# Reordering the prologue of a fused attention and feed-forward kernel: first loads, first scores and output-weight splits

## The reference

```
scale = 1/8
pp  = softmax(scale * p @ k^T) @ v         # 32 packed rows per head
x   = softmax(scale * q @ pp^T) @ pp       # back to 576 rows, heads side by side: [4608, 512]
xn  = x / rms(x) * rms_g
x   = (silu(xn @ w_gate) * (xn @ w_val)) @ moe_w_out     # inner size 1536
y   = (((x @ w1) * (x @ w2)) @ w3) @ w_out               # inner size 1024, all fp32
```

## Time and profile before

| | |
|---|---|
| runs | 1411.97, 1412.69, 1413.43 us (median 1412.69) |
| profiled execution | 1412.07 us, of which the span of the core is 1410.3 us |
| TensorE matmuls | 1386.3 us busy, 98% of the span |
| VectorE, ScalarE, GpSimd | 605.7, 406.9, 141.4 us busy |
| chain that ended last | PE 95%, DVE 3%, ACT 1%, issue 1% |
| granted TensorE clock | mean 0.999 |

### The profile page before, as it was taken

How to read it: one execution, slowest core, us unless ns; L and a number is a source line. 1 busy time by engine, 2 the same in 40 slices (tenths; PEclk the granted TensorE clock), 3 DMA queues, 4 the chain that set the end, 5 groups by cost and what they waited for, 6 DMA issues and landing times.

```text
span 1410.3 us, 22634 instructions
## 1 busy us (share of the span) xinstructions
PE 1386.3 (98%) x9688; PEld 1194.8 (85%) x9688; DVE 605.7 (43%) x1095; ACT 406.9 (29%) x803; POOL 141.4 (10%) x137
## 2 busy tenths in 40 slices
PE   7989999999999999999999999999999999999999
PEld 5679899898898998988989988888888888888887
DVE  3657556565565565655655632212212111212111
ACT  4253342433423424334233422111111111111111
POOL 0100100001001000010012030220202020202000
PEclk9999999999999999999999999999999999999999
DMA  9882451533424515323024130101011010100000
GB/s 332 233 314 82 129 163 41 196 106 93 165 86 128 163 39 197 107 92 131 18 69 167 47 107 0 60 0 60 0 60 45 16 60 0 60 0 30 0 30 30
DMA packets 59155, 129.13 MB, mean 92 GB/s; under 512 B 3504, under 2 KB 12720, under 8 KB 57264
## 3 DMA queue, kind: packets, MB, share of 16 engines
q1 hardware_dynamic: 59056, 127.70, 27.6%
HBM read 106.69 MB, written 20.99 MB: 91 GB/s over the span
## 4 chain that ended last, share of the span: by engine, by line
PE 95%; DVE 3%; ACT 1%; issue 1%; DMA 0%; SPq 0%; DVEq 0%; ACTq 0%
PE psum L586 9%; PE psum L584 9%; PE psum L585 9%; PE psum L546 8%; PE psum L565 7%; PE psum L567 7%; PE psum L566 7%; PE psum L547 7%; PE psum L548 7%; PE psum L606 5%; PE psum L605 5%; PE psum L604 5%; PE psum L513 3%; PE psum L500 1%; PE psum L526 1%; PE psum L467 1%
## 5 line engine op out<-in xcount | busy, mean ns | idle before, releaser
L546 PE MATMUL psum<-a_hi,m_hi 128*128 128x288 f32 x768 | 240.7, 313 | 0.4
L565 PE MATMUL psum<-g_hh,wo_hi 128*128 128x288 f32 x768 | 227.4, 296 | 4.5 <-DVE g_res L921 2.6
L547 PE MATMUL psum<-a_lo,m_hi 128*128 128x288 f32 x768 | 226.7, 295 | 0.0
L548 PE MATMUL psum<-a_hi,m_lo 128*128 128x288 f32 x768 | 226.3, 295 | 0.0
L567 PE MATMUL psum<-g_hh,wo_lo 128*128 128x288 f32 x768 | 226.0, 294 | 0.0
L566 PE MATMUL psum<-g_hl,wo_hi 128*128 128x288 f32 x768 | 225.9, 294 | 0.0
L1012 DVE TENSOR_TENSOR b_h<-b_s,psum 128x512 f32<-128x512 f32 x72 | 49.5, 688 | 408.9 <-PE psum L586 408.9
L584 PE MATMUL psum<-xh,w_hi 128*128 128x512 f32 x576 | 224.1, 389 | 0.0
L585 PE MATMUL psum<-xl,w_hi 128*128 128x512 f32 x576 | 224.1, 389 | 0.0
L586 PE MATMUL psum<-xh,w_lo 128*128 128x512 f32 x576 | 224.1, 389 | 0.0
L546 PEld LDWEIGHTS psum<-a_hi,m_hi 128*128 128x128 f32 x768 | 144.4, 188 | 50.6 <-issue 46.6
(11 more groups left out here) (109 smaller groups left out, 1737.2 us busy)
## 6 DMA issues: line engine op xcount, KB each, us to landing
w_in<-in_w_gate SPq DMA_DIRECT2D x24, 1024.0 KB, 5.3
w_in<-in_w_val SPq DMA_DIRECT2D x24, 1024.0 KB, 5.3
kT<-in_kT SPq DMA_DIRECT2D x8, 1152.0 KB, 7.7
v_sb<-in_v SPq DMA_DIRECT2D x8, 1152.0 KB, 7.2
qT<-in_qT SPq DMA_DIRECT2D x16, 576.0 KB, 3.8
y_scratch<-g_res SPq DMA_DIRECT2D x16, 576.0 KB, 3.2
x_raw<-y_scratch SPq DMA_DIRECT2D x9, 1024.0 KB, 7.6
out<-b_res SPq DMA_DIRECT2D x8, 1024.0 KB, 5.2
```

The costliest lines, as they stand in the source:

```text
L546: nc.tensor.matmul(in_ps[which], hi, a2_hi[:, t, par, :], start=par == 0, stop=False)
L547: nc.tensor.matmul(in_ps[which], hi, a2_lo[:, t, par, :], start=False, stop=False)
L548: last = nc.tensor.matmul(in_ps[which], lo, a2_hi[:, t, par, :], start=False, stop=par == 1)
L565: nc.tensor.matmul(out_ps[m], hi, hh[:], start=f == 0, stop=False)
```

## The change

All of it concerns the prologue and the first steps of the main loop:
1. Loads: the first piece of w_out and w3 is one chunk instead of two and is loaded ahead of pT and kT of batch 0 (pieces of 1, 1, 2, 2, 2 chunks). The second half of w3 comes ahead of batch 1's pT and kT. The output weights come in pieces of 1, 3, 4, 4 chunks, and `store_wf(1)` stands after the second piece.
2. TensorE: fuse(0,0) ahead of the first scores; fuse(0,1) and fuse(0,2) ahead of both AT items, which stand side by side.
3. S1(0,1) and AT(0,1) write banks 0 and 1 and don't wait for the item before them to be copied out.
4. The lo parts of w_out (eight subtractions) move from VectorE to GpSimd.
5. S1(1,0) and S1(1,1) move from the end of the prologue to places after fuse(0,7) and fuse(1,1).
6. ScalarE's and VectorE's orders follow: ScalarE copies both AT items before fuse_split(0,3); VectorE does fuse_split(0,2) before sums1, `wf_evict(0)` after fuse_split(1,2), and `wf_evict(1)` after M(0,3).

```diff
 FIRST_ITEMS = [("S1", 0, 0), ("S1", 0, 1), ("AT", 0, 0), ("AT", 0, 1), ("PV", 0, 0), ("PT", 0, 0), ("S2", 0, 0), ("S2", 0, 1),
-               ("Z", 0, 0), ("Z", 0, 1), ("SS", 0, 0), ("M", 0, 0), ("M", 0, 1), ("M", 0, 2), ("M", 0, 3),
-               ("S1", 1, 0), ("S1", 1, 1)]
+               ("S1", 1, 0), ("Z", 0, 0), ("S1", 1, 1), ("Z", 0, 1), ("SS", 0, 0), ("M", 0, 0), ("M", 0, 1), ("M", 0, 2), ("M", 0, 3)]
+FUSE_LOADS = [slice(0, 1), slice(1, 2), slice(2, 4), slice(4, 6), slice(6, 8)]
+WO_LOADS = [slice(0, 1), slice(1, 4), slice(4, 8), slice(8, 12)]
...
+def first_bank(kind, a, part):
+
+    return 0 if kind in ("S1", "AT") and (a, part) == (0, 1) else 6
...
+            load_fuse(0, 0)
             load_kp(0)
-            load_fuse(0, 0)
             load_fuse(0, 1)
+            load_fuse(0, 2)
             load_v(0)
-            load_fuse(0, 2)
             load_fuse(0, 3)
+            load_fuse(0, 4)
             load_q(0, 0)
             sp.dma_start(gcol[:], g_d).then_inc(g_loaded, 16)
             load_q(0, 1)
+            for i in range(len(FUSE_LOADS)):
+                load_fuse(1, i)
             load_kp(1)
-            for i in range(4):
-                load_fuse(1, i)
...
-            for i in range(3):
-                rows = slice(4 * i, 4 * i + 4)
+            for i, rows in enumerate(WO_LOADS):
                 sp.dma_start(wo_raw[:, rows, :], wo_v[:, rows, :]).then_inc(wo_loaded[i], 16)
-                if i == 0:
+                if i == 1:
                     store_wf(1)
...
+            for c in range(FC2):
+                pool.wait_ge(wout_hi_ready, c + 1)
+                nc.gpsimd.tensor_tensor(wout_lo[:, c, :], wout_raw[:, c, :], wout_hi[:, c, :].bitcast(F32),
+                                        ALU.subtract).then_inc(wout_lo_ready, 1)
...
             pe.wait_ge(const_ready, 3)
+            fuse(0, 0)
             item("S1", 0, 0)
             item("S1", 0, 1)
-            fuse(0, 0)
             fuse(0, 1)
+            fuse(0, 2)
             item("AT", 0, 0)
-            fuse(0, 2)
             item("AT", 0, 1)
             fuse(0, 3)
...
             fuse(0, 7)
+            item("S1", 1, 0)
             fuse(1, 0)
             item("Z", 0, 0)
             fuse(1, 1)
+            item("S1", 1, 1)
             fuse(1, 2)
...
-            item("S1", 1, 0)
-            item("S1", 1, 1)
             for b in range(B):
...
+            fuse_split(0, 0)
             item("S1", 0, 0)
             item("S1", 0, 1)
-            fuse_split(0, 0)
             fuse_split(0, 1)
             exp1(0, 0)
             exp1(0, 1)
             fuse_split(0, 2)
             item("AT", 0, 0)
+            item("AT", 0, 1)
             fuse_split(0, 3)
-            item("AT", 0, 1)
             fuse_split(0, 4)
...
-            fuse_split(1, 0)
-            fuse_split(1, 1)
+            for c in range(3):
+                fuse_split(1, c)
             wf_evict(0)
+            item("S1", 1, 0)
             exp2(0, 1)
-            for c in range(2, FC2):
+            fuse_split(1, 3)
+            fuse_split(1, 4)
+            item("S1", 1, 1)
+            for c in range(5, FC2):
                 fuse_split(1, c)
...
             act.wait_ge(wf_stored[0], 16)
-            item("S1", 1, 0)
-            item("S1", 1, 1)
             wo_split(0)
...
             def fuse_split(half, c):
-                if half == 0:
-                    dve.wait_ge(wout_hi_ready, c + 1)
-                    nc.vector.tensor_tensor(wout_lo[:, c, :], wout_raw[:, c, :], wout_hi[:, c, :].bitcast(F32),
-                                            ALU.subtract).then_inc(wout_lo_ready, 1)
...
             fuse_split(0, 1)
+            fuse_split(0, 2)
             sums1(0)
-            for c in range(2, 7):
+            for c in range(3, 7):
                 fuse_split(0, c)
...
-            wf_evict(0)
             item("Z", 0, 0)
             fuse_split(1, 2)
+            wf_evict(0)
             fuse_split(1, 3)
...
             a2_split(0, 0)
+            item("M", 0, 3)
             wf_evict(1)
-            item("M", 0, 3)
             wo_split(0)
```

More of the change, by code:

```diff
@@ L65, in item_numbers, with load_of @@
     return number
+def load_of(loads, c):
+    return next(i for i, rows in enumerate(loads) if c < rows.stop)
+def first_bank(kind, a, part):
+    return 0 if kind in ("S1", "AT") and (a, part) == (0, 1) else 6
 def before(b, t, f):
@@ L191, in build @@
         w_in_loaded = [sem(f"w_in_loaded{i}") for i in range(W_BUFS)]
-        wout_loaded = [sem(f"wout_loaded{i}") for i in range(4)]
-        w3_loaded = [[sem(f"w3_loaded{h}{i}") for i in range(4)] for h in range(2)]
+        wout_loaded = [sem(f"wout_loaded{i}") for i in range(len(FUSE_LOADS))]
+        w3_loaded = [[sem(f"w3_loaded{h}{i}") for i in range(len(FUSE_LOADS))] for h in range(2)]
         wout_hi_ready, wout_lo_ready = sem("wout_hi_ready"), sem("wout_lo_ready")
         w3_hi_ready, w3_lo_ready = sem("w3_hi_ready"), sem("w3_lo_ready")
-        wo_loaded = [sem(f"wo_loaded{i}") for i in range(3)]
+        wo_loaded = [sem(f"wo_loaded{i}") for i in range(len(WO_LOADS))]
         fuse_done, wf_act, wf_dve, wf_stored = sem("fuse_done"), sem("wf_act"), sem("wf_dve"), [sem(f"wf_stored{i}") for i in range(2)]
@@ L295, in load_fuse @@
             def load_fuse(half, i):
-                rows = slice(2 * i, 2 * i + 2)
+                rows = FUSE_LOADS[i]
                 if half == 0:
@@ L458, in item @@
                 n = number[kind, a, part]
-                if n:
+                bank = first_bank(kind, a, part)
+                if bank == 0:
+                    n -= 1
+                if n > 0:
                     pe.wait_ge(xy_free, n)
@@ L466, in item @@
                             rows, cols = slice(DH * par, DH * (par + 1)), slice(NP * c, NP * (c + 1))
-                            last = nc.tensor.matmul(xy[par][cols, 0:HALF], pT[rows, cols], kT[rows, c, HALF * part:HALF * (part + 1)],
+                            last = nc.tensor.matmul(psum[cols, bank + par, 0:HALF], pT[rows, cols], kT[rows, c, HALF * part:HALF * (part + 1)],
                                                     start=True, stop=True)
@@ L471, in item @@
                     for j in range(NT):
-                        last = nc.tensor.transpose(xy[j // 3][0:TP, j % 3 * P:(j % 3 + 1) * P], sc[:, part, TP * j:TP * (j + 1)], ident[:])
+                        last = nc.tensor.transpose(psum[0:TP, bank + j // 3, j % 3 * P:(j % 3 + 1) * P], sc[:, part, TP * j:TP * (j + 1)], ident[:])
                 if kind == "PV":
@@ L660, in item @@
                     full(act, "S1", a, part)
-                    nc.scalar.copy(sc[:, :, HALF * part:HALF * (part + 1)], psum[:, 6:8, 0:HALF]).then_inc(xy_free, 1)
+                    bank = first_bank(kind, a, part)
+                    nc.scalar.copy(sc[:, :, HALF * part:HALF * (part + 1)], psum[:, bank:bank + 2, 0:HALF]).then_inc(xy_free, 1)
                 if kind == "AT":
                     full(act, "AT", a, part)
-                    nc.scalar.copy(a1T[:, part, :].rearrange("p (a n) -> p a n", a=2), psum[0:TP, 6:8, 0:3 * P]).then_inc(xy_free, 1)
+                    bank = first_bank(kind, a, part)
+                    nc.scalar.copy(a1T[:, part, :].rearrange("p (a n) -> p a n", a=2), psum[0:TP, bank:bank + 2, 0:3 * P]).then_inc(xy_free, 1)
                 if kind == "PV":
@@ L699, in fuse_split @@
                 if half == 0:
-                    act.wait_ge(wout_loaded[c // 2], 16)
+                    act.wait_ge(wout_loaded[load_of(FUSE_LOADS, c)], 16)
                     nc.scalar.copy(wout_hi[:, c, :], wout_raw[:, c, :]).then_inc(wout_hi_ready, 1)
-                act.wait_ge(w3_loaded[half][c // 2], 16)
+                act.wait_ge(w3_loaded[half][load_of(FUSE_LOADS, c)], 16)
                 nc.scalar.copy(w3_hi[half][:, c, :], w3_raw[half][:, c, :]).then_inc(w3_hi_ready, 1)
@@ L706, in wo_split @@
                 act.wait_ge(fuse_done, 2)
-                act.wait_ge(wo_loaded[f // 4], 16)
+                act.wait_ge(wo_loaded[load_of(WO_LOADS, f)], 16)
                 nc.scalar.copy(wo_hi[:, f, :], wo_raw[:, f, :]).then_inc(wo_hi_ready, 1)
```

## The result

| | before | after |
|---|---|---|
| runs | 20, 1411.86 to 1413.43 us | 20, 1413.58 to 1418.76 us |
| median | 1412.46 us | 1416.72 us |
| ratio, after to before | | 1.0028, 95% interval 1.0021 to 1.0035 |
| profiled execution | 1412.07, span 1410.3 | 1413.70, span 1411.9 |
| start of outof(0) in it | 84.88 | 86.16 |

The changed kernel is slower by 0.28%, 4.3 us in the median. Two things stand out. The profiled execution is only 1.6 us slower than before, and it is one of the fastest of its kind: the kernel before spreads over 1.6 us, the changed one over 5.2. So the result has two halves, what the profile shows in every execution, and what differs between them.

A forecast was written before the change was run, and what follows sets the result against it. PE is busy 98% of the span, so only its waits and slow stretches can be won. Front +3.5, middle -1.35, loop start -3.3 sum to -1.15; one clock fall of 1.4 makes +0.3: 1413.0 us, range 1408.5 to 1416.5.

The forecast's parts named there:

- step 1: First loads: w_out chunk 0 lands at 4.2 us, w3 chunk 0 at 5.1, kT 1.35 later than before.
- step 2: Front splits: POOL and DVE subtractions exclude each other, one turn each; the exposed pair takes 2.0 us instead of 1.35.
- The case where POOL keeps two in a row: W_out chunks 3 and 4, ready at once: POOL does both subtractions first, making DVE's w3_lo(3) 1.3 us later; kept for the range.
- step 3: Front up to PV: first step 5.9 us earlier, PV 3.2 late; with chunk 5's exposed split, +3.5 us.
- Gap 1: PE's wait for w3_lo(1) ahead of fuse(0,1): 3.3 us.
- gap 2: PE's new wait for w3_lo ahead of fuse(0,3), behind the two AT items: 3.75 us.
- step 4: Middle, up to M(0,3): waits for w3_lo and w3b_lo vanish, -2.65; batch 1's two S1 come in, +1.3; sum -1.35 us.
- step 5: Loop start, M(0,3) to outof(0): S1 waits go, outof(0) then waits for DVE's g_hl; -3.3 us.
- the clock: Slower rival: long slow start or fall at gap 1, plus falls at gap 2 and outof(0); 1415 to 1417 us, chance 0.20.
- Exclusion doesn't bite: Faster rival: POOL and DVE overlap in the front, PV only 0.95 late; sum -3.7, 1409.0 us, chance 0.22.
- the start isn't earlier: Rival: first small pieces land at 6 instead of 5.1, times to PV move by 0.9; +1.2, 1413.9 us, chance 0.08.
- It does nothing: Rival: new gaps repay the earlier start, no clock fall; -1.15, 1411.5 us, chance 0.5 together with the main case.

The follow-up runs named there:

- the kernel with fillers: Changed kernel plus extra matmuls after into(0) and into(1) and ahead of fuse(0,1) and fuse(0,3), filling PE's waits: 1412.17 us, ratio 0.9999.
- maxima moved: Kernel with the front as before and the rest of the change, plus maxima and bias of batch 1's first scores moved ahead of M(0,0): 1409.71 us.
- the old front: Changed kernel with loads, order, banks and splits up to PV as in the kernel before: 1409.36 us, ratio 0.9979.

## Why the prediction was right or wrong

I had forecast 1413.0 with 1408.5 to 1416.5, and gave slower by over 0.2% a chance of 0.17, the smallest. The measured ratio is just that, and the median of 1416.72 lies at the end of the range, 0.2 beyond it. For the profiled execution, 0.6 under the median before, the same sum gave 1412.3, and it took 1413.70. That it came so near is partly luck: loads that were 1.0 earlier than reckoned covered most of the 1.4 by which the middle failed. For the median the side was wrong.

**First loads (step 1): earlier than reckoned.** ACT's first cast started at 3.35, not 4.2; w_out chunk 0 landed 2.6 us after its issue. fuse(0,0) started at 5.97 instead of 7.0.

**Exclusion (step 2): right.** w3_lo took 1.36 in the median beside POOL and 0.68 without. At chunks 3 and 4 the two subtractions of each engine took 2.96 on POOL and 3.04 on DVE together, one turn each, as I took it. The Trainium skill ("SBUF — State Buffer", "Who interferes with whom") states that the second blocks until the first finishes, which this agrees with; that each waits for one at most was my reading, since it doesn't say whose turn comes next. The case where POOL keeps two in a row didn't occur in the front.

**Front (step 3): right but for the clock.** Gap 1 was 3.33 (3.3 forecast), the wait for chunk 2 0.48 (0.3), gap 2 3.34 (3.75). PE's slow start was longer than reckoned: the matmuls of fuse(0,0) are 0.43 apart up to 10.37, and the step took 5.03 instead of 4.3. With no fall PV starts at 29.24 in the kernel with fillers; 30.1 less the 1.0 of the loads is 29.1.

**Middle (step 4): this step failed.** I forecast -1.35. PV moved by +4.34 (26.89 to 31.23), and M(0,3) by +4.64 (72.92 to 77.56), so this stretch took 0.3 more. Of that, 0.2 is the exposed split of chunk 5 (fuse(0,5) starts 0.24 behind PT, 0.03 before), forecast as 0.3 and counted in the front; the middle itself gave nothing. The waits named there did vanish, but S1(1,0) needs the banks of the second S2, whose transposition VectorE does only behind normalize2 and a split: PE stood for 0.94, 1.1 from issue to issue; the other 0.3 is spread over small gaps and my reading of them. I had counted what was taken from VectorE's chain and not asked whom the moved item now waits for.

**Into the loop (step 5): right in the waits.** From M(0,3) to outof(0) it was 11.96 and is 8.60: -3.36, -3.3 forecast. outof(0) was to start at 83.7 without a fall and at 85.3 with the one in gap 2; less 1.0 for the loads and 1.4 later for the middle that is 84.1 and 85.7. It started at 86.16 with that fall, and at 84.14 in the kernel with fillers, which has none: apart from the middle and the loads, the sum of the waits holds.

**The clock: right in kind, wrong in size.** I took one fall in the front at 1.4, and put 0.3 on the loop start, in the rival alone. At the loop start the fall lasted 6.8 us in four of the profiles, not 3.4, and so reaches full-speed work that no wait covers: 2.3 to 2.5 us are lost behind outof(0) in three of them, 1.0 to 1.4 in the fourth (maxima moved). The kernel before fell there too, but for 3.4 us, and nothing is lost behind its outof(0) (1410.3 - 84.88 = 1325.4). What it lost ahead of it, where into(0) ran at half clock and ScalarE waited 0.5 for its result, wasn't measured. The rival "the clock" was the mechanism that decided, at 4.5 us in the median and not at the rare end: a chance of 0.20 was too small for gaps that I had myself found as long as the one that made it fall before. "Exclusion doesn't bite" fell, "the start isn't earlier" too. "It does nothing" (1411.5, no fall) comes near the kernel with fillers (1412.17); no execution of the changed kernel was under 1413.5.

## What to carry to other kernels

When an item is moved on TensorE, write down for each other engine what now stands ahead of the split or copy that the next large step needs; here two copies in a row ahead of one split cost more than a load order and two banks had won, and moving each split one place up made 1416.7 into 1406. A wait as long as one behind which this kernel's clock was seen to fall has to be priced with the fall and with its spread, and one profile isn't enough to see it: compare the spread of the runs first. Filling a wait with harmless matmuls separates the two costs in one more kernel. And when a wait is gone, look for what comes behind it: with the splits ahead it was the landing of a load that had had time to spare until then.

## What the runs showed that I had not expected

The length of the fall isn't fixed. At the loop start it was 3.4 us in the kernel before and in two variants (the old front, the splits ahead), 6.8 in four (the changed kernel's second profile, lo parts on VectorE, AT apart, maxima moved), and there was none in the changed kernel's first profile, for nearly the same code around it. Why it is one or the other is open. In the front it was 3.4 us each time but once: behind gap 1 it lasted 6.8 in the kernel with only the loop start filled.

PE's slow start varies as well, and the granted clock in the profile doesn't show it. Of two kernels with the same first step, both starting at 5.99, one had its matmuls 0.43 apart up to 8.69 and 0.23 from 8.99 on, the other 0.43 up to 10.82, all twelve; both have 1.00 as granted clock. In the changed kernel this passes through: with its front order the first scores started at 10.51 to 11.43 in four profiles (unfilled twice, and the two with fillers), and gap 1 ended 4.5 to 4.8 us behind them, at 15.1 to 16.2. With the splits ahead it doesn't: there the landing of w3 chunk 2 sets PV, and the 1.5 us between these two kernels (22.77 and 24.31) are the 1.55 between their casts of it (14.35 and 15.90). These 1.5 us are more than the 0.4 of the edit under test.
